# A recurrent attention and two MLP layers on one core: one decay table copied in reverse, r and k decayed apart, and three batches moved in the order

## The reference

```
for t in range(768):                      # attention, state (B, H, 48, 48)
    cur   = outer(u * k[t], v[t])
    y[t]  = r[t] @ (state + cur)
    state = w * state + outer(k[t], v[t])
x = y as (3072, 384)
h = x @ w_in;  g = h * sigmoid(1.702 * h);       x = g @ w_out      # layer 0, 384 -> 2048 -> 384
h = x @ w_in2; g = h * tanh(softplus(h));        x = g @ w_out2     # layer 1
```

## Time and profile before

| | |
|---|---|
| time, median of 3 runs | 891.69 us (889.41 to 892.55) |
| profiled execution, whole | 891.01 us |
| its span | 889.2 us |
| mean granted clock of TensorE in it | 0.998 |
| TensorE busy | 881.2 us (99%), 5162 instructions |
| TensorE weight loads busy | 729.9 us (82%) |
| VectorE, ScalarE, GpSimd busy | 332.8, 290.8, 161.2 us |

### The profile page before, as it was taken

The page is one execution under the profiler, slowest core; times in us unless marked ns, Lnnn a source line. Parts: engine busy times, 40 slices in busy tenths (PEclk is TensorE's granted clock), DMA queues, the critical chain, the costliest instruction groups (busy, mean ns, idle before and its releaser), DMA issues.

```text
span 889.2 us, 12941 instructions
## 1 busy us (share of the span) xinstructions
PE 881.2 (99%) x5162; PEld 729.9 (82%) x5162; DVE 332.8 (37%) x466; ACT 290.8 (33%) x536; POOL 161.2 (18%) x126
## 2 busy tenths in 40 slices
PE   8999999999999999999999999999999999999998
PEld 8899888887888878878888888888888888888886
DVE  6876436434453553533244222222222221221111
ACT  3534332232223222222454422322322322322322
POOL 5969604222250422220000000000000000000000
PEclk9999999999999999999999999999999999999999
DMA  9464213212330422221430000000000000000000
GB/s 260 138 202 127 73 47 80 77 49 63 104 85 12 110 68 63 63 64 37 158 107 18 1 0 1 36 1 1 35 1 1 36 1 0 36 1 1 36 0 36
DMA packets 38250, 49.54 MB, mean 56 GB/s; under 512 B 6288, under 2 KB 30736, under 8 KB 38192
## 3 DMA queue, kind: packets, MB, share of 16 engines
q1 hardware_dynamic: 37248, 48.52, 18.6%
q10 hardware_dynamic: 944, 0.20, 0.1%
HBM read 36.11 MB, written 4.72 MB: 46 GB/s over the span
## 4 chain that ended last, share of the span: by engine, by line
PE 97%; DVE 2%; issue 0%; ACT 0%; POOL 0%; POOLq 0%; DVEq 0%
PE h L967 45%; PE acc L996 44%; PE a_bank L857 3%; PE pair L890 2%; PE pair L903 1%; PE a_bank L915 1%; DVE g_lo L762 0%; PE pair L1009 0%; PE acc L1009 0%; DVE mid L698 0%; PE pair L876 0%; PE pair L883 0%; DVE arena L678 0%; DVE act L721 0%; DVE act L704 0%
## 5 line engine op out<-in xcount | busy, mean ns | idle before, releaser
L762 DVE TENSOR_TENSOR g_lo<-act,g_hi 128x512 fp32r<-128x512 f32 (+1 forms) x202 | 176.9, 876 | 492.1 <-ACT g_hi L566 491.9
L967 PE MATMUL h<-xs,win_hi 128*128 128x512 f32 (+1 forms) x1212 | 340.0, 383 | 0.1
L967 PEld LDWEIGHTS h<-xs,win_hi 128*128 128x128 f32 x1212 | 219.8, 188 | 44.9 <-issue 1.0
L563 ACT ACTIVATE act<-h 128x512 f32<-128x512 f32 (+1 forms) x202 | 116.4, 576 | 266.4 <-PE h L967 254.2
L566 ACT ACTIVATE g_hi<-h 128x512 fp32r<-128x512 f32 (+1 forms) x202 | 116.6, 577 | 252.5 <-PE acc L996 252.4
L996 PE MATMUL acc<-g_hi,wout_hi 128*128 128x512 f32 (+1 forms) x606 | 167.8, 379 | 0.0
L996 PE MATMUL acc<-g_hi,wout_lo 128*128 128x512 f32 (+1 forms) x606 | 167.7, 379 | 0.0
L996 PE MATMUL acc<-g_lo,wout_hi 128*128 128x512 f32 (+1 forms) x606 | 167.7, 378 | 0.0
L967 PE MATMUL h<-xs,win_lo 128*128 128x512 f32 (+1 forms) x606 | 164.3, 379 | 0.0
L967 PEld LDWEIGHTS h<-xs,win_lo 128*128 128x128 f32 x606 | 111.1, 188 | 22.0
L996 PEld LDWEIGHTS acc<-g_hi,wout_hi 128*128 128x128 f32 x606 | 111.2, 188 | 21.7
(11 more groups left out here) (90 smaller groups left out, 389.3 us busy)
## 6 DMA issues: line engine op xcount, KB each, us to landing
arena<-in_rk SPq DMA_DIRECT2D x46, 192.0 KB, 3.5
mid<-in_wts SPq DMA_DIRECT2D x16, 384.0 KB, 7.1
arena<-in_wts SPq DMA_DIRECT2D x16, 384.0 KB, 3.4
xs<-xt SPq DMA_DIRECT2D x117, 48.0 KB, 2.0
arena<-in_k SPq DMA_DIRECT2D x22, 192.0 KB, 3.7
arena<-in_r SPq DMA_DIRECT2D x22, 192.0 KB, 4.0
arena<-in_v SPq DMA_DIRECT2D x22, 192.0 KB, 3.8
out<-mid SPq DMA_DIRECT2D x5, 768.0 KB, 3.3
```

Of the source, the lines that this page charges most:

```text
L563: act.activation(act1[:, g % 2, 0:c1 - c0], h_bank[g % 2][:, 0:c1 - c0], GATES[layer])
L762: dve.tensor_tensor(g_lo[:, g % 2, cols], act1[:, g % 2, cols], f32(g_hi[:, g % 2, cols]), ALU.subtract).then_inc(glo_done, 1)
L967: ins = pe.matmul(hb, w[:, f, kd, :], x_part(lo, par, kd)[:, c0:c1], start=i + kd == 0, stop=i == 2 and kd == KD - 1)
```

## The change

Six things are done.

1. The doubling chain on VectorE makes the first table alone. ScalarE copies it in reverse into the second (semaphore `flipped`). GpSimd's `decay_t`, which reads the second table, waits for that.
2. Batches 0 and 1: r and k are multiplied apart, in four instructions of 112x512: r of 0, r of 1, then, after the wait for `flipped`, k of 0, k of 1. `r_first` counts four up for them, and all waits on it are raised by two.
3. WARM goes from 20 to 14; four products are put between the two early_sums, and one in place of three stands ahead of the first unit.
4. The first unit's high-part products wait for x_hi of both batches only, its last three for x_lo.
5. decay_rk(2) moves on VectorE ahead of split_g(1); VectorE's two low_out stand one behind and one between, where they stood behind the two x_lo; on ScalarE one weight split moves ahead of x_hi(0); on GpSimd low_in(3) and low_out(2) go ahead of the wait for u and bonus(2).
6. LATE goes from 8 to 9; scores of 4 and 5 go from steps 9, 12 to 10, 13, their bursts from 11, 14 to 12, 15. Scores 6 and 7 stay at 16, 19 and their bursts at 18, 21.

```diff
-WARM = 20
+WARM = 14
-LATE = 8
+LATE = 9
-SCORES = [{1: 2, 4: 3, 9: 4, 12: 5, 16: 6, 19: 7}] + ...
-BURST = [{3: 2, 6: 3, 11: 4, 14: 5, 18: 6, 21: 7}] + ...
+SCORES = [{1: 2, 4: 3, 10: 4, 13: 5, 16: 6, 19: 7}] + ...
+BURST = [{3: 2, 6: 3, 12: 4, 15: 5, 18: 6, 21: 7}] + ...
...
             def product(n):
-                pool.wait_ge(r_first, n + 1)
+                pool.wait_ge(r_first, EARLY + n + 1)
...
             pool.wait_ge(chain, LOGS)
+            pool.wait_ge(flipped, 1)
...
             for f in range(3):
                 low_in(f)
+            low_in(3)
+            low_out(2)
             pool.wait_ge(u_in, 16)
             bonus(2)
-            low_in(3)
-            low_out(2)
...
             act.preload_act_table(GATES[0])
+            act.wait_ge(runs, LOGS)
+            act.activation(decay[:, 1], decay[:, 0, :, ::-1], ACT.Copy).then_inc(flipped, 1)
...
             split_out(0, 0)
             split_out(0, 1)
+            split_in(0, 3)
             x_hi_part(0)
-            split_in(0, 3)
...
-                    dve.tensor_copy(decay[:, 1, :, CH - 1], powers[:, LOGS - 2, 1, :]).then_inc(runs, 1)
             for n in range(LOGS - 1):
                 m = 1 << n
-                dve.wait_ge(runs, 2 * n + 2)
+                dve.wait_ge(runs, n + 1)
                 dve.tensor_tensor(decay[:, 0, :, m:2 * m], ...).then_inc(runs, 1)
-                dve.tensor_tensor(decay[:, 1, :, CH - 2 * m:CH - m], ...).then_inc(runs, 1)
             dve.wait_ge(chain, LOGS)
-            dve.wait_ge(runs, 2 * LOGS)
+            dve.wait_ge(runs, LOGS)
+            def decay_half(n, a):
+                dve.wait_ge(rk_in[n], 32)
+                dve.tensor_tensor(first[n].rk[:, a], first[n].rk[:, a], decay[:, a], ALU.mult).then_inc(r_first, 1)
...
+            for n in range(EARLY):
+                decay_half(n, 0)
+            dve.wait_ge(flipped, 1)
+            for n in range(EARLY):
+                decay_half(n, 1)
             dve.wait_ge(pattern, 4)
-            decay_rk(0)
-            decay_rk(1)
             select(0)
             select(1)
             diagonal(0)
             diagonal(1)
+            low_out(0)
             x_lo_part(0)
+            low_out(1)
             x_lo_part(1)
-            low_out(0)
-            low_out(1)
             split_g(0)
+            decay_rk(2)
...
-                    if t == 0 and s == 0:
-                        decay_rk(2)
...
                 if n < B:
-                    pe.wait_ge(r_first, n + 1)
+                    pe.wait_ge(r_first, EARLY + n + 1)
...
                         else:
-                            pe.wait_ge(xlo_done, b + 1)
+                            pe.wait_ge(xhi_done, b + 1)
                 for i, (w, lo) in enumerate(((win_hi, 0), (win_lo, 0), (win_hi, 1))):
                     if f == 0 and lo and layer:
                         pe.wait_ge(m_lo, (t - NT) * KD + KD)
+                    elif f == 0 and lo and t == 0:
+                        pe.wait_ge(xlo_done, c1 // CH)
...
             early_sums(0)
+            keep_warm(acc[0], 4)
             early_sums(1)
             keep_warm(acc[0], 2)
             inside(0)
             inside(1)
             decay_rows()
-            keep_warm(acc[1], 3)
+            keep_warm(acc[1], 1)
```

More of the change, by code:

```diff
@@ L48 @@
 BASE = [sum(len(u) for u in UNITS[:t]) for t in range(2 * NT + 1)]
-SCORES = [{1: 2, 4: 3, 9: 4, 12: 5, 16: 6, 19: 7}] + [{3 * b: (t + 1) * B + b for b in range(B)} for t in range(1, NT - 1)] + [{}] * (NT + 1)
-BURST = [{3: 2, 6: 3, 11: 4, 14: 5, 18: 6, 21: 7}] + [{3 * b + 2: (t + 1) * B + b for b in range(B)} for t in range(1, NT - 1)] + [{}] * (NT + 1)
+SCORES = [{1: 2, 4: 3, 10: 4, 13: 5, 16: 6, 19: 7}] + [{3 * b: (t + 1) * B + b for b in range(B)} for t in range(1, NT - 1)] + [{}] * (NT + 1)
+BURST = [{3: 2, 6: 3, 12: 4, 15: 5, 18: 6, 21: 7}] + [{3 * b + 2: (t + 1) * B + b for b in range(B)} for t in range(1, NT - 1)] + [{}] * (NT + 1)
 IN_AT = [{f - 4: f for f in range(4, HALF)} | {f + 2: f for f in range(HALF, NF)}] + [{}] * (2 * NT - 1)
@@ L182, in mlp_rwkv_program @@
         runs = sem("runs")
+        flipped = sem("flipped")
         dsrc = sem("dsrc")
@@ L664, in _ @@
                     dve.tensor_copy(decay[:, 0, :, 0], powers[:, LOGS - 2, 1, :]).then_inc(runs, 1)
-                    dve.tensor_copy(decay[:, 1, :, CH - 1], powers[:, LOGS - 2, 1, :]).then_inc(runs, 1)
             for n in range(LOGS - 1):
                 m = 1 << n
-                dve.wait_ge(runs, 2 * n + 2)
+                dve.wait_ge(runs, n + 1)
                 dve.tensor_tensor(decay[:, 0, :, m:2 * m], decay[:, 0, :, 0:m], wide(powers[:, n, 0, :], m), ALU.mult).then_inc(runs, 1)
-                dve.tensor_tensor(decay[:, 1, :, CH - 2 * m:CH - m], decay[:, 1, :, CH - m:CH], wide(powers[:, n, 0, :], m),
-                                  ALU.mult).then_inc(runs, 1)
             dve.wait_ge(chain, LOGS)
-            dve.wait_ge(runs, 2 * LOGS)
+            dve.wait_ge(runs, LOGS)
+            def decay_half(n, a):
+                dve.wait_ge(rk_in[n], 32)
+                dve.tensor_tensor(first[n].rk[:, a], first[n].rk[:, a], decay[:, a], ALU.mult).then_inc(r_first, 1)
             def decay_rk(n):
```

## The result

The changed kernel takes 896.66 us (median of 20 runs, 889.15 to 897.63), the kernel before on the same chip 891.60 (20 runs, 889.41 to 894.58): ratio 1.0044, 95% interval 1.0026 to 1.0061. The forecast was 889.3, with a range up to 893.2. The executions come in kinds, told apart by TensorE's mean granted clock: four at 889.2 to 891.6 us with 0.998 to 1.000; six at 892.9 to 896.0 with 0.992 to 0.996; ten at 897.3 to 897.6, all with 0.990. The profiled one took 895.15 at 0.992, span 893.3 (before: 889.2). One execution of a later kernel (974.81 us, clock 0.85, in e12_apart_warm26_step4_undone) was in the chip's slower state and is left out of its times.

A forecast was written before the change was run, and what follows sets the result against it. TensorE, busy 881.2 of 889.2 us, was taken to bound the kernel. -1.8 - 1.1 - 0.9 + 1.75 = -2.05 gave 889.0 from 891.01 and 889.6 from the median; forecast 889.3, own range 888.0 to 890.6, full range 886.8 to 893.2.

The forecast's parts named there:

- Bounds: TensorE, busy 881.2 of 889.2 us: gains only from an earlier first unit or removing two waits, 1.3 and 0.9 us.
- Step 1: Decay tables at the start: first ready at 6.4, ScalarE's reverse copy takes 0.6, second at 7.0; backward read hidden.
- Step 2: r and k apart on VectorE: batch 1's second load gates at 8.25, so scores(0) starts at 9.6, against 9.48.
- Step 3: Warm products at the start: TensorE idles 1.7 us, inside runs at 2.4 GHz, first unit at 18.7, not 20.5: -1.8.
- the clock still falls: Rival, chance 0.14: clock falls before inside(0) despite the warm products; first unit at 20.9, +0.4; total 890.9.
- The rival of the late rise: Rival, chance 0.12: clock rises after the warm stretch, the start runs at 1.2 GHz, first unit 3 us later; 893.7.
- Step 4: Batch 2 decayed sooner on VectorE: of the 1.3 us wait at scores(2), 0.2 stays: -1.1.
- Step 5: LATE and batches 4 and 5 one step later: L698's wait goes, -0.9; new wait at scores(6), +1.75 (0.9 to 2.5).
- scores(7) at no cost: Within tile 0: scores(7) waits for batch 6, but three steps, two of them 512 wide, lie there: 0.
- keep up with an earlier TensorE at no cost: GpSimd's moved low_in(3) and low_out(2) fill waiting time: 0; otherwise up to 1.8 of the start's gain is lost.

The follow-up runs named there:

- e12_apart_warm26_step4_undone: Changed kernel with WARM 26, scores and bursts of batches 6 and 7 one step later, decay_rk(2) back behind split_g(1): 889.90 us, 0.9976 to the kernel before.
- e17_apart_warm14: Changed kernel, WARM 14 kept, with scores and bursts of batches 6 and 7 one step later: 893.66 us, 1.0016 to the kernel before.
- e18_after_third: Changed kernel unchanged, run on the same chip beside the WARM 14 version with scores apart: 896.70 us, 1.0044 to the kernel before.
- e3: Changed kernel, WARM 14, with r and k decayed batch by batch (r0, k0, r1, k1) and waits to match: 892.37 us, 1.0004 to the kernel before.
- e6: Changed kernel with WARM 26 in place of 14: 890.06 us, 0.9977 to the kernel before.
- e8: Changed kernel with WARM 20 and scores and bursts of batches 6 and 7 one step later: 887.96 us (4 runs), 0.9956 to the kernel before.
- e10: Changed kernel with WARM 26 and scores and bursts of batches 6 and 7 one step later: 890.18 us, 0.9973 to the kernel before.
- e16: Changed kernel with WARM 20 and scores and bursts of batches 6 and 7 one step later, run again: 888.79 us (11 runs), 0.9973 to the kernel before.
- e1: Changed kernel with WARM back at 20, nothing else: 890.38 us, 0.9977 to the kernel before.
- e2: Kernel before with WARM 14 instead of 20, nothing else: 891.05 us, 0.9986 to the kernel before.
- e5: Kernel before with decay_rk(1) ahead of decay_rk(0), scores(0) and product(0) waiting for both: 892.96 us, 1.0012 to the kernel before.
- e11: Changed kernel with WARM 26, scores and bursts of batches 6 and 7 one step later, without the four warm products: 889.43 us, 0.9967 to the kernel before.
- e4_warm20_old_tables: Changed kernel with WARM 20 and LATE, SCORES and BURST as in the kernel before: 889.64 us, 0.9976 to the kernel before.
- e13_after_look: Changed kernel unchanged, one execution for a profile: 897.97 us, clock 0.990.
- e14_after_look: Changed kernel unchanged, a second single execution for a profile: 897.64 us, clock 0.990.
- e9_after_again: Changed kernel unchanged, run again: 894.87 us (10 runs), 1.0023 to the kernel before.
- e15_after_look: Changed kernel unchanged, a third single execution for a profile: 894.59 us, clock 0.994.

## Why the prediction was wrong

**Bounds.** Right: only the start, the waits and the clock moved the time.

**Step 1** held: the reverse copy takes 0.63 us (0.6 taken) and hides behind the load. ScalarE's timeline:
```profile
6.24 0.63 ACT L593 ACTIVATE arena<-arena 112x512 f32<-112x512 f32 x1 [2.61 <-DVE arena L674]
```
**Step 2** held. Scores(0) at 9.66 (9.6 forecast); VectorE stands 1.17 us (1.2) for the second rk load. Its timeline:
```profile
6.45 0.69 DVE L681 TENSOR_TENSOR arena<-arena 112x512 f32<-112x512 f32 x1 [0.24 <-DMA arena<-in_rk]
8.31 1.89 DVE L681 TENSOR_TENSOR arena<-arena 112x512 f32<-112x512 f32 x3 [1.17 <-DMA arena<-in_rk]
```
**Step 3 is the step that failed**: "I expect it at 2.4 GHz, since warm products now lie between the two groups of single columns". The pause was seen and priced as idle time alone; behind it the clock fell before the first scores had ended, and everything to inside(1) ran at 1.2 GHz. The first unit came at 25.44 instead of 18.7: 6.7 us, more than the whole miss of this profile. The pause was also longer than said. WARM 14 was said to end near 7.92, which is where the fourteenth pair of the earlier trace rows starts; it ends at 8.14. In the changed kernel's profile the warm products ended at 7.54, since the clock rose sooner, and 1.7 us became 2.1. The nineteen profiles taken after the prediction, set beside each other:

| pause, us | kernel | clock fell by the end of scores(1) |
|---|---|---|
| 2.6, 2.5, 2.4, 2.3, 2.2, 2.1 | scores apart with WARM 14; load by ScalarE; changed kernel (four) | yes, each |
| 2.0, 1.8, 1.8 | old tables; changed kernel (two) | yes, each |
| 1.6, 1.3, 1.1 | before with pause; batch by batch (ahead of scores(1)); before with WARM 14 | no |
| 1.0, 1.0, 0.1, 0 (four) | the others with WARM 20 or 26 | no |

In e17_apart_warm14 and e18_after_third (pauses of 2.6 and 2.4) the clock fell inside the pause; in the other seven it fell 0.1 to 1.6 us after scores(0) had begun. The table goes by pauses as they came, and no run sets the pause alone to a chosen length. What speaks for it as the cause is that the same kernel lost its fall by warm products alone, that 20 of them didn't help where the pause was 2.0 or 2.5, and that 14 did no harm where it was 1.1 or 1.3.

The moment at which the warm pairs shorten moved between executions: over all profiles the first pair of full speed starts at 5.05 to 8.16 us, over the six of the changed kernel at 5.93 to 7.69, and with it moved the end of the warm products (7.22 to 8.08 in those six). The load's landing moved too (8.23 to 8.69 there). Both set the pause; that the kind at 889 is the one with a short pause is argued from this and not shown. The Trainium skill ("TensorE: Matmul & The Clock Gate", the part on the clock gate) says that the point differs between runs of one kernel; these runs agree.

That four warm products between the sums hold the clock was a sound idea, but for a clock that is still up. In the changed kernel they ran at half themselves, 2.01 us for the eight instructions of L850 at 14.75, against 1.09 with WARM 20. Of the seven profiles that have the four and no fall at the start, six keep the clock at 1.00 through both insides (e3, e6, e8, e10, e12, e16) and one loses it at 14.8 (e1). All four profiles without them (the kernel before, e2, e5, e11) lose it between 13.4 and 15.4.

The rival "the clock still falls" named the mechanism with 0.14, but ended the fall at 18 as in the earlier trace rows and began it behind scores: it gave 890.9. The rival of the late rise (893.7) came nearest the time, by another cause: the pairs do shorten in each profile. Its terms add up to 5.7 - 1.8 = 3.9 us for the first unit, and not to the 3 that it says.

**Step 4**: the wait at scores(2) is gone in every profile of the changed kernel, as forecast. That step 4 is what takes it away, and is worth 1.1 us, isn't shown: with the step undone the wait stayed away, and the time was the same.

**Step 5**: L698's wait went (-0.9), and a new wait for the state came, of 0.7 to 2.1 us (1.75 forecast, 0.9 to 2.5 its range). With the old tables, too, scores(6) waited 0.76 us (e4_warm20_old_tables, e5_before_pause), so the full step between burst(5) and scores(6) was no sure cover. Its place was half wrong. I had scores(7) at no cost, with "three steps, two of them 512 wide"; one step lies between burst(6) and scores(7), and burst(6) didn't move while burst(5) did, so the moves of batch 5 came late for x_hi(6). ScalarE's timeline, x_hi(5) and x_hi(6):
```profile
75.58 0.60 ACT L545 ACTIVATE xt<-pair 112x512 fp32r<-112x512 f32 x1 [0.96 <-DMA xs<-xt]
...
87.97 0.60 ACT L545 ACTIVATE xt<-pair 112x512 fp32r<-112x512 f32 x1 [3.79 <-DMA xs<-xt]
```
Whether scores(6) or scores(7) waits goes with when the ten moves of batch 4 land: x_hi(5) starts 1.5 us behind their last issue here, and 3.2 in e13_after_look. And a wait was priced at its length only; one of 1.8 to 2.1 us can lower the clock as well, +1.7.

**GpSimd** was taken to keep up with an earlier TensorE at no cost (0 in step 4). Where the first unit starts at 19 to 20, win_lo is late by up to 0.9 us.

Open: why waits of about 1.8 us lowered the clock in some executions (e14_after_look, e2_before_warm14) and not in others (e3_by_batch, e9_after_again, e15_after_look); what sets the landing time of the moves; and what holding the clock through the insides is worth in time, since without the four warm products nothing was lost.

## What to carry to other kernels

An idle stretch of the bounding engine has two prices: its length, and, if the granted clock falls behind it, half of the stretch that follows. Look at the clock row behind every pause that a change lengthens, and ask what fills it. Moving one of several equally spaced steps squeezes the next pair, so go through the distances of all of them. Where executions of one kernel differ by 8 us, sort them by granted clock before asking what a change did.

## What was not expected of the hardware

- Falls of the clock were of unequal length: 3.4 us at 81 to 84 us, among the units, but 10.2 or 13.6 us at the start (9.9 to 23.6 in the changed kernel's profile), with TensorE busy in all of it.
- A load of 192 KB issued 1.1 us sooner, on a second queue, landed 0.9 us later (9.24 against 8.30).
- ScalarE copies 112x512 in reverse in 0.63 us; an operation of the same shape that reads forward takes 0.60.
- One operation of VectorE on the same shape took 3.41 and 1.67 us, 10 us apart in the profile after. Its timeline, then GpSimd's:
```profile
70.80 3.41 DVE L729 COPY_PREDICATED arena<-arena 128x1024 f32<-128x1024 uint32 x1
...
81.16 1.67 DVE L729 COPY_PREDICATED arena<-arena 128x1024 f32<-128x1024 uint32 x1
```
```profile
70.64 2.40 POOL L455 TENSOR_TENSOR arena<-arena 112x1024 f32<-112x1024 f32 x1
...
81.60 3.45 POOL L455 TENSOR_TENSOR arena<-arena 112x1024 f32<-112x1024 f32 x1
```
The slow one starts 0.16 us behind GpSimd's and ends 1.2 us after GpSimd's has ended; in the second pair VectorE starts first, and it is GpSimd's that takes 3.45 us for 2.40. So the one that starts second seems to stand until the first is done. decay_rk(2) shows the same: 2.03 us where a GpSimd operation had started 0.24 us before it, 1.22 where it started first (e12_apart_warm26_step4_undone). No run here moves such a pair apart on purpose.
